# One program part for attention and experts, each crossing with its own wait, and two blocks of the first products ahead of the ranks

## The reference, cut to what matters

```python
# attention: 4 batches x 8 heads, 576 positions, head size 64
scores = scale * q @ k.T
thresh = max(scores) - tau;  scores[scores < thresh] = -1e9
attn = exp(scores - max) / (sum + 1e-9);  out = attn @ v
# experts: x is [2304, 512], 8 experts, hidden 1024
logits = (x / |x|) @ (emb / |emb|).T / moe_tau
expert_idx = argmax(logits);  gate_w = softmax(logits)[expert_idx]
for e in range(8):  out[mask_e] = gate_w * (relu(x[mask_e] @ w1[e]) @ w2[e])
# feed forward: 2304 tokens, hidden 1536
g = x @ w_gate;  y = (g * sigmoid(g) * (x @ w_val)) @ w_out
```

## Time and profile before

| | us |
|---|---|
| median of 3 runs | 1096.19 (1094.42 to 1096.23) |
| the profiled execution | 1094.56 |
| its span, first to last instruction | 1093.0 |
| PE busy in the span | 1081.7 |
| DVE / ACT / POOL busy | 547.7 / 499.1 / 228.1 |
| mean granted TensorE clock | 0.998 |

### The profile page before, as it was taken

One profiled execution on the slowest core, in us unless ns is written; L12 is line 12 of the kernel. 1 busy time (PEld: TensorE's weight loads), 2 busy tenths in 40 slices (PEclk: granted clock), 3 DMA queues, 4 the chain that ended last, 5 costly groups with the idle time before them and its releaser, 6 DMA issues.

```text
span 1093.0 us, 19307 instructions
## 1 busy us (share of the span) xinstructions
PE 1081.7 (99%) x6765; PEld 1000.5 (92%) x6766; DVE 547.7 (50%) x953; ACT 499.1 (46%) x881; POOL 228.1 (21%) x221
## 2 busy tenths in 40 slices
PE   9999999999999899999999999999999999999998
PEld 8999999999999688888888889999999999999997
DVE  6777677767878764555543544322223223223222
ACT  7678777877776653554443442221211212212212
POOL 6433653564331111122211100010100100100101
PEclk9999999999999999999999999999999999999999
DMA  7323324262201566565534322010010100100000
GB/s 248 127 87 112 124 91 152 73 207 82 87 23 66 192 215 195 192 202 202 193 122 138 116 98 68 1 59 1 20 39 1 60 1 1 59 1 1 30 1 29
DMA packets 36992, 101.38 MB, mean 93 GB/s; under 512 B 3048, under 2 KB 5736, under 8 KB 36912
## 3 DMA queue, kind: packets, MB, share of 16 engines
q1 hardware_dynamic: 30848, 78.95, 21.3%
q0 software_dynamic: 5904, 21.26, 5.8%
q10 hardware_dynamic: 160, 0.08, 0.0%
HBM read 85.32 MB, written 14.95 MB: 92 GB/s over the span
## 4 chain that ended last, share of the span: by engine, by line
PE 64%; DVE 1%; issue 1%; ACT 1%; ACTq 0%; POOL 0%; DVEq 0%
PE hb L1360 14%; PE hp L1305 10%; PE yp L1330 10%; PE hp L1378 9%; PE gp L1360 7%; PE vp L1360 7%; PE xb L1378 5%; PE hb L1323 2%; PE xb L1293 1%; PE yp L1345 1%; ACT w_hi L1486 0%; ACTq L1151 0%; DVE w_lo L1493 0%; DVE ht_lo L1640 0%; PE yp L1418 0%
## 5 line engine op out<-in xcount | busy, mean ns | idle before, releaser
L388 PE MATMUL o_ps<-v_in,prob_t 128*128 128x74 f32 (+1 forms) x1440 | 181.0, 273 | 0.0
L388 PEld LDWEIGHTS o_ps<-v_in,prob_t 128*128 128x128 f32 x1440 | 174.0, 192 | 0.2 <-ACT prob_t L470 0.2
L594 DVE TENSOR_REDUCE neg_max<-scores 128x1 f32<-128x576 f32 x144 | 109.1, 758 | 85.6 <-PE scores L347 84.5
L470 ACT ACTIVATE prob_t<-scores 128x640 f32<-128x640 f32 x144 | 101.9, 708 | 75.1 <-PE scores L357 74.4
L605 DVE SCALAR_TENSOR_TENSOR expo<-scores,thresh,expo 128x576 f32<-128x576 f32 x144 | 116.4, 808 | 0.5 <-DVE thresh L597 0.5
L463 ACT ACTIVATE expo<-scores,neg_max 128x576 f32<-128x576 f32 x144 | 107.3, 745 | 0.4 <-DVE neg_max L594 0.4
L357 PE MATMUL scores<-ident,expo 128*128 128x128 f32 x720 | 102.2, 273 | 0.4 <-DVE expo L605 0.2
L347 PE MATMUL scores<-kt_hi,qt 128*128 128x288 f32 x320 | 102.1, 336 | 0.3
L1280 POOL DMA_INDIRECT out<-stage,out_row x18 | 17.7, 983 | 398.4 <-ACT stage L1552 395.1
L1360 PE MATMUL hb<-f_xt_hi,w_hi 128*128 128x384 f32 x288 | 97.5, 339 | 0.0
L1360 PE MATMUL hb<-f_xt_hi,w_lo 128*128 128x384 f32 x288 | 96.7, 336 | 0.0
(11 more groups left out here) (309 smaller groups left out, 2417.3 us busy)
## 6 DMA issues: line engine op xcount, KB each, us to landing
stage<-in_moe_w SPq DMA_DIRECT2D x18, 1024.0 KB, 5.5
stage_more<-in_moe_w SPq DMA_DIRECT2D x14, 1024.0 KB, 8.1
q_raw<-in_q SPq DMA_DIRECT2D x15, 640.0 KB, 7.2
k_raw<-in_k SPq DMA_DIRECT2D x15, 576.0 KB, 5.0
v_in<-in_v SPq DMA_DIRECT2D x16, 370.0 KB, 3.0
ys<-y_out POOLq DMA_DIRECT2D x21, 256.5 KB, 3.1
vt_in<-in_vt SPq DMA_DIRECT2D x16, 320.0 KB, 2.9
stage<-in_moe_w_val SPq DMA_DIRECT2D x3, 1024.0 KB, 5.3
```

Source lines behind the costliest of these rows:

```text
L388: last = nc.tensor.matmul(dst, prob_t[:, g % 3, 128 * c:128 * (c + 1)], src, start=(c == 0), stop=(c == KEY_CHUNKS - 1))
L470: nc.scalar.activation(prob_t[:, g % 3, :], scores[g % 3][:].rearrange("p a c -> p (a c)")[:, 0:KEY_CHUNKS * 128], ACT.Copy).then_inc(s_pt ...
L594: V.tensor_reduce(neg_max[:, t:t + 1], scores[g % 3][:, :, 0:HALF], mybir.AxisListType.XY, ALU.max, negate=True).then_inc(s_max, 1)
```

## The change

It opens one block in `build` and gives it to both functions, with one allocator of semaphores for both. `attention` returns the semaphores that the experts have to look at (`Attended`), and each place of the experts where an engine touches what attention leaves or uses gets a wait on one of them. DVE's last addition to the logits gets a semaphore. On PE two blocks of the first slot's products, not one, stand ahead of the ranks.

```diff
-def attention(nc, q, k, v, ...
+def attention(nc, block, sem, q, k, v, ...
...
+        s_logits = sem("s_logits")
...
-        block = ctx.enter_context(nc.Block())
...
-            V.tensor_tensor(logit[:, TILES:2 * TILES, :], logit[:, TILES:2 * TILES, :], own[:], ALU.add)
+            V.tensor_tensor(logit[:, TILES:2 * TILES, :], logit[:, TILES:2 * TILES, :], own[:], ALU.add).then_inc(s_logits, 1)
...
+        return Attended(s_x, s_o_sb, s_logits, s_xt_hi, s_xt_lo, s_sq)
...
-        block = ctx.enter_context(nc.Block(no_gpsimd_drain=True))
...
         @block.sync
         def _(sp):
+            sp.wait_ge(attended.x, PAIRS - 1)
+            sp.wait_ge(attended.o_sb, STEPS)
             store_rows(sp, x_rows, x_sb, 1, slice(LAST_FEATURES, FEAT), s_xrows)
             for c in range(CHUNKS):
+                if c < 2:
+                    sp.wait_ge(s_wlo, c + 3)
...
             pe.wait_ge(s_wlo, CHUNKS)
-            hidden_products(w_in, range(0, 1))
+            pe.wait_ge(attended.xt_hi, 2)
+            pe.wait_ge(attended.xt_lo, 2)
+            hidden_products(w_in, range(0, 2))
+            pe.wait_ge(attended.o_sb, STEPS - 1)
             pe.wait_ge(s_oh, 1)
...
-            hidden_products(w_in, range(1, KC)).then_inc(s_h, 1)
+            hidden_products(w_in, range(2, KC)).then_inc(s_h, 1)
             keep_warm(WARM[0])
             hidden_t(0)
             keep_warm(WARM[1])
+            pe.wait_ge(attended.o_sb, STEPS)
             pe.wait_ge(s_row, 1)
...
+            act.wait_ge(attended.x, PAIRS - 1)
+            act.wait_ge(attended.o_sb, STEPS)
             for t in range(TILES, T - 2):
                 square(t)
...
             hidden_hi(0)
+            act.wait_ge(attended.squares, TILES)
             act.wait_ge(s_sq, TILES)
...
+            dve.wait_ge(attended.logits, 1)
             step(V.tensor_reduce(best[:, late], logit[:, late, :], AX, ALU.max))
...
+        block = ctx.enter_context(nc.Block(no_gpsimd_drain=True))
+        attended = attention(nc, block, sem, q, k, v, ...
+        experts_and_feed_forward(nc, block, sem, attended, x_rows, ...
```

More of the change, by code:

```diff
@@ L3 @@
 from contextlib import ExitStack
+from dataclasses import dataclass
 import concourse.bass as bass
@@ L140, with attention @@
 FILLERS = (3, 4, 5)
-def attention(nc, q, k, v, vt, emb, emb_t, w1, w2, x_rows, weights, ident, consts, early, token_of, xt, logit,
+def attention(nc, block, sem, q, k, v, vt, emb, emb_t, w1, w2, x_rows, weights, ident, consts, early, token_of, xt, logit,
               squares, s_xrows):
@@ L155, in sb @@
             return ctx.enter_context(nc.sbuf_tensor(name, shape, dt))
-        def sem(name):
-            return ctx.enter_context(nc.semaphore(name))
         above = [weights.spare]
@@ L860, in _ @@
             normalise(PAIRS - 2)
+        return Attended(s_x, s_o_sb, s_logits, s_xt_hi, s_xt_lo, s_sq)
+@dataclass
+class Attended:
+    x: object
+    o_sb: object
+    logits: object
+    xt_hi: object
+    xt_lo: object
+    squares: object
 BEHIND_ROWS = 480
@@ L1015, with experts_and_feed_forward @@
 WARM = (3, 2, 7)
-def experts_and_feed_forward(nc, x_rows, ys_dram, out, w1, w2, wg, wv, wo, weights, slot_tab, token_of, xt, ident,
+def experts_and_feed_forward(nc, block, sem, attended, x_rows, ys_dram, out, w1, w2, wg, wv, wo, weights, slot_tab, token_of, xt, ident,
                              consts, early, s_xrows):
     with ExitStack() as ctx:
-        def sem(name):
-            return ctx.enter_context(nc.semaphore(name))
         at = [nc.sbuf_base]
@@ L1832, in build, with sem @@
         consts, early = Consts(nc, weights), Early(nc, weights)
-        attention(nc, q, k, v, vt, emb, emb_t, w1, w2, x_rows, weights, ident, consts, early, token_of, xt,
+        sems = ctx.enter_context(ExitStack())
+        def sem(name):
+            return sems.enter_context(nc.semaphore(name))
+        block = ctx.enter_context(nc.Block(no_gpsimd_drain=True))
+        attended = attention(nc, block, sem, q, k, v, vt, emb, emb_t, w1, w2, x_rows, weights, ident, consts, early, token_of, xt,
                   consts.logit, consts.squares, s_xrows)
-        experts_and_feed_forward(nc, x_rows, ys, out, w1, w2, w_gate, w_val, w_out, weights, slot_tab, token_of, xt, ident,
+        experts_and_feed_forward(nc, block, sem, attended, x_rows, ys, out, w1, w2, w_gate, w_val, w_out, weights, slot_tab, token_of, xt, ident,
                                  consts, early, s_xrows)
```

## The result

The changed kernel takes 1098.12 us (median of 14 runs, 1095.89 to 1098.64) against 1096.22 us (14 runs, 1094.19 to 1097.03): a ratio of 1.0023, 95% interval 1.0016 to 1.0030. The forecast was 1094.0, and 1098.1 was the figure of its rival C.

What follows compares the result with a forecast made beforehand. PE, busy 1081.7 of 1093.0 us, was taken as the bound, gains coming only from its waits or lowered clock; `hidden(1)` starting 2.2 us earlier took the median from 1096.19 to 1094.0, range 1092.2 to 1097.0.

Steps and rivals of the forecast that it cites:

- rival C: Slot 1's gather falls behind the weight chunks, gain gone, idle PE then costs 1.9 us at half clock: 1098.1; chance 0.16.
- the gather of slot 1 moves with `token_of`: issue 371.2, landing 3.7 us later: Slot 1's gather lands at 374.9; PE's output products meet it at 374.6, so `hidden(1)` starts at 379.0 instead of 381.24.
- The packet rule: DMA engines go round queues packet by packet, so the gather is only slowed a little and the sum stays 2.2 us.
- PE's first products, clock at 1.00: At the boundary, 12 products follow the last value product without idle time, 2.75 us from 359.69, at full clock.
- The ranks' result at 3.22 us behind (362.9): DVE's L1700, behind PE's 11 small rank matmuls, starts at 362.9 instead of 364.80, 1.9 us earlier.
- relu at 7.06 us behind (366.75), held by ACT's squares: ACT starts relu at 366.75 instead of 369.44, once its squares end at 366.7; PE idles about 1.1 us.
- L1729 at 10.3 us behind (370.0): DVE's L1729, behind the inverse, starts at 370.0 instead of 372.29, 2.3 us earlier, without waiting for the inverse.
- The gain on the path, 2.2 us: L1729 and `hidden(1)` both start 2.2 to 2.3 us earlier, unpriced waits of 0.1 included; the lower was taken.
- Rival A: The clock's fall at the boundary isn't in every execution, so the change is worth only 0.6 us: 1095.6; chance 0.17.
- Rival B: Stepping into the new body costs PE or DVE as much as the barrier, and the clock still falls: 1095.3; chance 0.12.
- SP's chunks 0 and 1 late for ACT, at nothing: Two chunk loads behind SP's stores, wanted by ACT at 371.7, keep under 1 us of cover; costed at nothing.
- The second block ahead of the ranks: PE runs 12 products ahead of the ranks, 12 instead of 18 behind; relu still waits for ACT's squares until 366.7.

Runs made afterwards that it cites:

- experiment 5: Changed kernel with chunks 2 and 3 also held on SP until DVE's second `ht_lo` is done: 1094.51 us against 1094.92, ratio 0.9994.
- a5_fill: Changed kernel plus 14 matmuls that nobody reads ahead of the transposes of slot 1: 1096.06 us against 1094.92, ratio 1.0008.
- a1_hold: Changed kernel with chunks 2 and 3 held on SP until slot 1's gather has landed: 1094.05 us against 1095.99, ratio 0.9983.
- a2_one_block: Changed kernel with one block of products ahead of the ranks instead of two, no hold: 1093.77 us against 1095.99, ratio 0.9987.
- b4_fill_barrier: Kernel before, barrier kept, plus 8 matmuls that nobody reads behind PE's last value product: 1094.63 us against 1096.63, ratio 0.9981.
- a9_gates_first: Changed kernel, one block, chunks held, slot 1's rows converted first, DVE's second weight-chunk split put behind the gates: 1097.01 us against 1096.63, ratio 1.0002.
- a4_gap_c26: Changed kernel with chunks 2 and 3 also held on SP until DVE's step 26: 1094.73 us against 1094.92, ratio 0.9994.

## Why the prediction was wrong

**The step that failed** is "the gather of slot 1 moves with `token_of`: issue 371.2, landing 3.7 us later". I carried the landing over from the trace of before as if it were a constant; it hangs on how far ahead of the chunks the gather is issued. I put that distance at 0.55 us. It was 0.25, and by experiment 5 even 0.51 costs 1.7 us of landing, of which 0.4 reach `hidden(1)` (20.09 against 19.69). The distance came out smaller because the gather gained 1.88 us (13.77 to 11.89 behind the last value product) and not 2.25, while the chunks gained 2.63 (14.77 to 12.14; forecast 2.7).

**Rival C had it**: the mechanism, its place and the clock. Its parts came out as 2.07 us for the late gather, where the working has 2.2, and 1.36 for the clock, where it has 1.9. That its total of 1098.1 agrees to 0.1 us is luck: its loss of 4.1 us was 3.4, and the gain that this eats was 1.9 and not 2.2; behind the last value product the trace is 1.3 us longer, not 1.9. What was wrong in C was its chance, 0.12 on the slower side. "The gather is still issued first" is no argument against it: in the changed kernel the gather is issued first and loses.

**The packet rule.** The DMA queues of the changed kernel from 375 to 377 us, with the gather out since 372.95:

```profile
q1 hardware_dynamic: 360, 0.74, 101.5%
```

No packet but SP's moved in 2 us. The Trainium skill (DMA: Bandwidth & Descriptors, Queues, rings and completion order) has each DMA engine go round the queues that it has work for, a packet at a time. These 2 us, and rows 9, don't look like that, but no run shows whether the gather's packets were ready by then. Once they move, both queues do. In a5_fill, with the same distance, the gather is issued at 371.51, so the same window lies 1.4 us later behind it:

```profile
q1 hardware_dynamic: 287, 0.56, 79.0%
q0 software_dynamic: 52, 0.20, 25.0%
```

In windows of 0.2 us the gather's first packet (q0) comes at 377.4 to 377.6 in the changed kernel, 4.5 us behind its issue, and at 375.0 to 375.2 in the kernel before, 1.6 us behind. From there to the landing it is 2.5 us and 2.1 us. So of the 3.3 us that the landing takes longer 2.9 lie before the first packet: the gather starts late, it is hardly slower once it runs. Why it starts late is not shown by any run.

Point by point:

- *PE's first products, clock at 1.00:* right. PE follows without idle time and the clock stays up.
- *The ranks' result at 3.22 us behind (362.9):* it was 3.62. The first part is 0.16 us of idle time on DVE behind L771, at the step into the second body, where the working has nothing but the 0.1 of waits; it is inside the bound of 0.31. The second is the way from the one-hot's end to L1719: 0.75 us by its row, where the working has 0.5 with those 0.1 in it (0.30 of ranks, 0.11 behind them). Before it was 5.11, so 1.5 of the forecast 1.9 us came.
- *relu at 7.06 us behind (366.75), held by ACT's squares:* right, 7.11.
- *L1729 at 10.3 us behind (370.0):* it was 10.72 (L1748). The shortfall is that of the ranks, nothing was added on the way.
- *The gain on the path, 2.2 us:* with the gather in time (a1_hold, a2_one_block) `hidden(1)` starts 19.69 and 19.67 us behind instead of 21.55, so 1.86 to 1.88. Of it 1.27 is the clock (b4_fill_barrier), the other 0.6 the barrier itself. Rival A's split was 1.7 and 0.6. In the profiled executions A is out: the four kernels with the barrier and an idle PE at it all show the fall. For a part of the others it is right. Over the experiments' four sets the kernel before ran 97 times; in 77 executions the mean granted clock is 0.998, as in its profile, and in 20 it is 1.000, a value that among the profiles only kernels without such a stretch show. All 14 executions of the changed kernel have 0.998, so its late gather brings the clock down each time, as far as this mean can tell.
- *Rival B:* out, by the clock in the changed kernel's trace.
- *SP's chunks 0 and 1 late for ACT, at nothing:* right. Issued at 365.2 and 365.8, they land 5.3 us later, by 371.1, and ACT takes them at 373.03 without a wait.
- *What follows `hidden(1)` moves with it:* right. From its start to the end of the span it is 733.3 - 21.55 = 711.8 us before, 734.6 - 23.12 = 711.5 after.
- *The second block ahead of the ranks* stood in my working as free, since relu waits for the squares anyway. It isn't: experiment 2 shows that the block lets ACT reach `norm`, and SP the chunks, 0.64 us earlier, and that is what the gather lacks.

Not tried: distances between 0.25 and 0.51 us, and how often each landing occurs at a given distance, since each kernel has one profiled execution.

## What to carry to other kernels

The time to landing in a trace belongs to the distance between the issues in that trace: when a change moves two queues by different amounts, work out that distance anew, and where the lead of a small, urgent gather over large loads shrinks, price the later landing as a term of its own (here a lead of 0.88 us was enough, 0.51 and 0.25 were not). A load that isn't urgent can be held by one wait on SP until the urgent one has landed; here that turned a loss of 0.23% into a gain of 0.17%, each against its own set of runs. And a faster engine off the path (ACT, by 0.64 us) can be the cause of a loss, through what it lets go.

## What the runs showed of the hardware that I had not expected

**The landing changes within a narrow range of the distance.** Between leads of 0.25 and 0.87 us it falls from 7.0 to 3.8 us, with one kernel between them (0.51 us, 5.4). From -0.71 to 0.25 us it stays at 6.9 to 7.1, and from 0.87 to 3.52 us at 3.8 to 3.2.

**PE's idle time and the clock.** By PE's own rows an idle 2.03 us stands at the fall to 0.50 in the kernel before, 3.32 us in the changed one and 3.87 us in a9_gates_first; 1.61 us (a2_one_block) and 1.74 us (a3_gap_hlo) brought none. But the barrier is in every execution of the kernel before, and in 20 of 97 the mean clock shows no fall. So the same code can give either.

**The start of the program differs between executions.** PE's last value product ends at 359.6 to 359.8 us in some profiled executions, at 361.1 to 361.5 in others and at 362.2 in three, in kernels whose code up to there does the same work. Of the five profiled kernels with the barrier four start early, of the nine without it two. The difference is there after 15 us. Timeline of PE in the kernel before and in a4_gap_c26, the products of the scores:

```profile
6.70 0.44 PE L347 MATMUL scores<-kt_lo,qt 128*128 128x288 f32 x1
...
7.80 0.29 PE L347 MATMUL scores<-kt_lo,qt 128*128 128x288 f32 x1
```

```profile
9.64 0.44 PE L344 MATMUL scores<-kt_lo,qt 128*128 128x288 f32 x1
...
14.51 0.30 PE L344 MATMUL scores<-kt_lo,qt 128*128 128x288 f32 x1
```

The same matmul takes 0.44 us at first and 0.29 later; the first short one comes at 7.8 us in one execution and at 14.5 in the other. The windows of both traces give a granted clock of 1.00 over this whole stretch, so they don't show the cause. The difference moves all that follows by up to 2.6 us, more than this change is worth, so single executions of two kernels can't be compared by their spans: that is why places stand here behind the last value product. The spread of the runs fits it: the kernel before's 77 executions with a mean clock of 0.998 fall into 20 from 1094.15 to 1095.04 us and 57 from 1095.67 to 1097.35, with none between, and PE's last value product ends 1.3 to 2.6 us apart in the two kinds of profile. So it mostly starts late, and its early profiles are the rarer kind. That the two groups are the two starts is argued and not shown.
